# Retention transposes of a 768-token kernel, made per head as products of 64 rows with half the identity

## The reference

```python
def _attn_ref(q, k, v):                      # B=2, H=8 heads, S=768, D=64
    gamma = 1.0 - 2.0 ** (-5.0 - np.arange(H))
    for t in range(S):
        state = gamma[None, :, None, None] * state + np.einsum('bhd,bhe->bhde', k[:, :, t], v[:, :, t])
        y[:, :, t] = scale * np.einsum('bhd,bhde->bhe', q[:, :, t], state)

def _moe_ref(x, U, V, w_ch1, w_ch2):         # x: (2, 768, 512), U: (768, 32), V: (32, 768)
    xt = x.transpose(0, 2, 1)
    h = xt @ U @ V
    u = x + h.transpose(0, 2, 1)
    ch = np.maximum(u @ w_ch1, 0.0) @ w_ch2
    return u + ch

def _moe2_ref(x, w_in, w_spatial, b_spatial, w_out):
    h = np.maximum(x @ w_in, 0.0)            # halves u and v; v is normalised over its channels
    v_s = np.einsum('ts,bsd->btd', w_spatial, v_n) + b_spatial[None, :, None]
    return (u * v_s) @ w_out
```

## Time and profile before

| what | value |
|---|---|
| time, median of 3 runs | 467.19 us (467.06 to 469.72) |
| the profiled execution's own time | 468.86 us |
| its span on the core | 466.9 us |
| TensorE busy | 458.2 us, 98% of the span |
| VectorE busy | 351.3 us, 75% |
| ScalarE busy | 253.6 us, 54% |
| granted TensorE clock, mean | 0.998 of full |

### The profile page before, as it was taken

One profiled execution on the slowest core, in us unless ns is written; L12 is line 12 of the kernel. 1 busy time (PEld: TensorE's weight loads), 2 busy tenths in 40 slices (PEclk: granted clock), 3 DMA queues, 4 the chain that ended last, 5 costly groups with the idle time before them and its releaser, 6 DMA issues.

```text
span 466.9 us, 8670 instructions
## 1 busy us (share of the span) xinstructions
PE 458.2 (98%) x3128; PEld 409.0 (88%) x3128; DVE 351.3 (75%) x772; ACT 253.6 (54%) x592; POOL 48.1 (10%) x52
## 2 busy tenths in 40 slices
PE   8899999999999999999999999999999999999995
PEld 4788898899999999888888999988888789999995
DVE  4788879977889978874855976765813998895783
ACT  1666756546667655843464655733523765564451
POOL 2178970000000000000100000000100001000000
PEclk9999999999999999999999999999999999999999
DMA  8989801433332343201220343302105002041003
GB/s 275 406 298 333 298 3 46 136 135 136 135 126 92 127 137 97 94 24 66 91 91 1 102 130 115 108 1 91 45 1 202 1 0 93 0 155 71 0 1 136
DMA packets 20889, 51.36 MB, mean 110 GB/s; under 512 B 1520, under 2 KB 3952, under 8 KB 19568
## 3 DMA queue, kind: packets, MB, share of 16 engines
q1 hardware_dynamic: 20432, 50.29, 31.3%
q10 hardware_dynamic: 416, 0.53, 0.4%
HBM read 47.66 MB, written 3.15 MB: 109 GB/s over the span
## 4 chain that ended last, share of the span: by engine, by line
PE 94%; DVE 2%; DMA 2%; ACT 1%; issue 0%; DVEq 0%
PE bank L1615 10%; PE bank L1613 10%; PE bank L1616 9%; PE bank L1594 9%; PE bank L1596 9%; PE bank L1597 8%; PE bank L1719 3%; PE bank L1721 3%; PE bank L1722 3%; PE bank L1460 3%; PE bank L1654 2%; PE bank L1653 2%; PE bank L1655 2%; PE bank L1505 2%; PE bank L1499 2%; PE bank L1737 2%
## 5 line engine op out<-in xcount | busy, mean ns | idle before, releaser
L1594 PE MATMUL bank<-bh,w1c 128*128 128x256 f32 x336 | 94.7, 282 | 0.3 <-DVE hl L1099 0.3
L1597 PE MATMUL bank<-bh,w1c 128*128 128x256 f32 x336 | 94.7, 282 | 0.0
L1596 PE MATMUL bank<-bl,w1c 128*128 128x256 f32 x336 | 94.6, 282 | 0.0
L1615 PE MATMUL bank<-hl,w2h 128*128 128x512 f32 x192 | 75.9, 395 | 0.0
L1613 PE MATMUL bank<-hh,w2h 128*128 128x512 f32 x192 | 75.8, 395 | 0.0
L1616 PE MATMUL bank<-hh,w2l 128*128 128x512 f32 x192 | 74.7, 389 | 0.0
L1594 PEld LDWEIGHTS bank<-bh,w1c 128*128 128x128 f32 x336 | 63.5, 189 | 7.0 <-issue 0.5
L1091 DVE TENSOR_TENSOR c<-bank,p 128x256 f32<-128x256 f32 x72 | 30.4, 423 | 51.1 <-PE bank L1597 29.8
L1596 PEld LDWEIGHTS bank<-bl,w1c 128*128 128x128 f32 x336 | 63.4, 189 | 5.4
L1597 PEld LDWEIGHTS bank<-bh,w1c 128*128 128x128 f32 x336 | 63.4, 189 | 0.0
L672 ACT ACTIVATE p<-bank 128x256 f32<-128x256 f32 x72 | 27.5, 381 | 45.4 <-PE bank L1597 44.3
(11 more groups left out here) (179 smaller groups left out, 948.3 us busy)
## 6 DMA issues: line engine op xcount, KB each, us to landing
w1raw<-w SPq DMA_DIRECT2D x24, 512.0 KB, 5.3
w2raw<-w SPq DMA_DIRECT2D x24, 512.0 KB, 4.1
att<-attn SPq DMA_DIRECT2D x7, 1152.0 KB, 7.8
att<-attn SPq DMA_DIRECT2D x10, 384.0 KB, 5.7
out_T<-stage SPq DMA_DIRECT2D x7, 384.0 KB, 2.5
wsp_raw<-w_sp SPq DMA_DIRECT2D x1, 2304.0 KB, 9.1
winraw<-w_in SPq DMA_DIRECT2D x4, 512.0 KB, 4.9
tab<-decay SPq DMA_DIRECT2D x7, 258.0 KB, 5.0
```

What stands on the lines that cost most here:

```text
L1594: mm(o, w1c[k][:, 0, q, s], bh[:, q, c, :], start=(opens and c == 0), stop=False, skip_group_check=True)
L1596: mm(o, w1c[k][:, 0, q, s], bl[:, q, c, :], start=False, stop=False, skip_group_check=True)
L1597: m = mm(o, w1c[k][:, 1, q, s], bh[:, q, c, :], start=False, stop=(c == 1), skip_group_check=True)
L1615: mm(ch_ps[c][:, :], w2h[h][:, s], hl[k][:, h, :], start=False, stop=False, skip_group_check=True)
```

## The change

For items 0 to 6 `turn(i, 0)` and `turn(i, 1)` are replaced by `turn_heads(i)`. It goes through the six chunks, and in each takes the heads one after the other: 64 rows of `xT` (one head's channels) as weights, 128 columns, times the 64 x 64 block of the identity on the same partitions. Head 0 writes `t_ps[0]` (bank 5), head 1 writes `t_ps[1]` (bank 7), 64 columns for each chunk. These are plain float32 products and not the instruction's transpose form. Both `t_done` signals come at the last chunk. The wait for `u_done` (bank 7 has been read by `u_add`) stands ahead of the first product. `xn_copy` and `xn_rest` take a head over all six chunks instead of three chunks with both heads. Item 7 keeps its transposes.

```diff
+        def t_part(i, g):
+            e = DH if i < NI - 1 else P
+            return t_ps[g][:, 0:GW].rearrange("p (c e) -> p c e", e=e)
+
+        def xn_part(t, i, g, s):
+            if i < NI - 1:
+                return t[:, :, s, g * DH:(g + 1) * DH]
+            return t[:, g * G:(g + 1) * G, s, :]
...
             def xn_copy(i, g):
                 act.wait_ge(t_done, 2 * i + g + 1)
-                nc.scalar.activation(xn[:, g * G:(g + 1) * G, 0, :],
-                                     t_ps[g][:, 0:GW].rearrange("p (c e) -> p c e", e=P),
-                                     ACT.Copy).then_inc(xn_hi, 1)
+                nc.scalar.activation(xn_part(xn, i, g, 0), t_part(i, g), ACT.Copy).then_inc(xn_hi, 1)
...
             def xn_rest(i, g):
                 dve.wait_ge(xn_hi, 2 * i + g + 1)
-                nc.vector.tensor_tensor(xn[:, g * G:(g + 1) * G, 1, :],
-                                        t_ps[g][:, 0:GW].rearrange("p (c e) -> p c e", e=P),
-                                        raw(xn)[:, g * G:(g + 1) * G, 0, :], ALU.subtract).then_inc(xn_lo, 1)
+                nc.vector.tensor_tensor(xn_part(xn, i, g, 1), t_part(i, g), xn_part(raw(xn), i, g, 0),
+                                        ALU.subtract).then_inc(xn_lo, 1)
...
+            def turn_heads(i):
+                pe.wait_ge(xt_done, 2 * i + 1)
+                pe.wait_ge(eye_loaded, 16)
+                if i:
+                    pe.wait_ge(u_done, 2 * i - 1)
+                for c in range(NC):
+                    if c == G:
+                        pe.wait_ge(xt_done, 2 * i + 2)
+                    for a in range(2):
+                        h = slice(a * DH, (a + 1) * DH)
+                        m = mm(t_ps[a][:, c * DH:(c + 1) * DH], xT[i % 2][h, c * P:(c + 1) * P], ident[h, h],
+                               start=True, stop=True)
+                        if c == NC - 1:
+                            m.then_inc(t_done, 1)
...
             for i in range(1, NI):
                 scores(i, 0)
-                turn(i - 1, 0)
-                turn(i - 1, 1)
+                turn_heads(i - 1)
```

## The result

| | before | after |
|---|---|---|
| median | 467.12 us | 471.97 us |
| lowest to highest | 466.68 to 469.72, 4 runs | 471.59 to 472.97, 4 runs |
| the profiled execution's own time | 468.86 us | 472.97 us |
| its span | 466.9 us | 470.5 us |

The ratio is 1.0102, with a 95% interval of 1.0088 to 1.0116: the change makes the kernel 4.85 us slower. The forecast was 3.6 us slower.

The account below looks back on a forecast made before the run. TensorE was taken to bound the kernel, busy throughout six iterations. 6 x (0.49 for the products + 0.09 for `down`) + 0.1 for `u_done` = 3.6 us on the 467.19 median gave 470.8 us, range 469.4 to 472.6.

Parts of the forecast that it names:

- The added step: TensorE, last scores to first kv: 12 product pairs at 0.112 us replace the transposes, 1.50 against 1.01, +0.49 us an iteration.
- kv's own border: TensorE's step from kv's last start (45.98) to the next step (46.13), taken as 0.15 us behind the new products.
- Rival (a): Products by heads on TensorE: the moving side sets the pace, 0.058 us a pair; 466.6 to 467.2 us, chance 0.12.
- (c): Rival: load and matmul of a pair don't overlap, 0.16 us a pair; 474.2 us, chance 0.04.
- The wait of `down`: TensorE's `down` waits for VectorE's rest, which ends 0.81 us later: +0.09 us of new wait an iteration.
- `u_done`: TensorE's earlier wait for VectorE's addition, with 0.18 us of cover less the signal's way: 0.1 us for all six iterations.
- the sentence on the length of `decay_q`: On VectorE ahead of `u_done`: where `decay_q` is long, DVE can be up to 0.1 us late.
- Item 0: Turned while TensorE waits for a mask copy anyway: nothing added; without that cover 0.49 us more.
- The forecast's own terms: From 6 x 0.46 without a new wait (469.9 us) to 6 x 0.7 (471.4 us); forecast's chance 0.70.
- rival (b): Chain copy, rest, `down` outgrows its cover: over 1% slower; with runs of 64 slowing copies, 472.2 us; chance 0.14.
- the range: Whole kernel: 469.4 to 472.6 us, leaving out (a), (c) and the far half of (b).
- The chance of 0.20 for over 1% slower: Whole kernel above 471.9 us: made up of (b), (c) and a little of the forecast.

Follow-up runs that it names:

- The first experiment: The changed kernel with each product by heads moving 128 columns instead of 64, same weights: 471.95 us, ratio 1.0098 to the kernel before.
- the second: The changed kernel with each product by heads taking only 64 of a chunk's 128 tokens as weights, bank 5 cleared at the start: 467.91 us, ratio 1.0014.
- transposes late: The kernel before with its transposes kept, but u_done awaited ahead of the first transpose and both t_done signals at the last: 467.73 us, ratio 1.0007.
- Two executions with quarters: The changed kernel with each product cut into two 64 x 64 ones: 470.53 us; the same with decay_q moved behind mask_a(i, 0): 471.33 us.

## Why the prediction was right, and where it was off

*The added step.* The prediction took 0.112 us for a pair, from the loads, and +0.49 for the interval. Measured is 0.111 to 0.112 and an interval of 1.48, +0.47. By the starts of the records the first of the eleven steps is 0.06 and not 0.112, and the border to kv 0.21 and not the 0.15 that was taken from kv's own border; the two cancel. Counted back from the ends of the records, as the prediction did with kv's 0.22, both are as predicted. The first experiment (moving columns doubled, nothing changes) and the second (weight columns halved, the step halves) show that the load is the cause. Rival (a) is dead, and (c) with it: load and moving side do overlap.

*The wait of `down`.* Predicted 0.09, measured 0.10 (0.30 against 0.20 at that border), and isolated with the transposes in place.

*`u_done`.* This is the term that was mis-sized. The prediction put 0.1 us on it for all six iterations together, from 0.18 us of cover and a DVE that "can be up to 0.1 late". It measured 1.2: 1.01 + 1.36 - 2 x 0.58. The profile counts 0.7 of that as waiting. It counts from the end of the last scores record, 0.27 us behind its start, where the first product otherwise starts after 0.11; that is another 0.3. The rest is that behind each of the two waits the 24 records take 1.28 instead of 1.18 us from first start to last. The step of the argument that failed is the sentence on the length of `decay_q`: it took the lengths of before, 0.83 to 1.2 us in these iterations, as fixed. They depend on how much of a GpSimd instruction is still to run when `decay_q` starts, and the change shifts VectorE against GpSimd, which is busy in nearly all of the last two iterations. Where item 6 is turned 0.46 us were left before and 1.19 after, and the 1.15 us of before became 1.86. With iterations of 7.38 and 7.42 us (transposes late, weights halved) the same `decay_q` took 0.94 and 0.87, and nothing waited for `u_done`; so the size of this term is in part chance. In the iteration that turns item 1 it was another lateness: `decay_q` has its 0.83 us but starts 0.24 us late, at 22.05, behind an idle time that the profile puts down to issue, so that the first addition ends at some 23.46, and the first product starts 0.47 us behind the scores instead of 0.11. Why `decay_q` starts late there stays open. With 1.2 instead of 0.1 the sum is 6 x 0.58 + 1.2 = 4.7, the measured value. The prediction calls itself wrong if `u_done` becomes a wait, and it became one: the added step and the wait of `down` held, this mechanism did not.

*Item 0* cost next to nothing, as said: its second half started on ScalarE's copy and the next scores still waited 0.32 us for the mask copy (0.66 before). From the first scores to these it is 16.64 - 13.62 = 3.02 us, against 2.95 before.

*The chances.* The forecast's own terms reached to 471.4 and the measured 471.97 lies beyond them, in what was left to rival (b), whose mechanism (the copies' chain growing through runs of 64) did not happen: two copies take 0.87 us, two rests 1.02, as before. That the range held the time, in the room of a rival that did not happen, is luck. The chance of 0.20 for over 1% slower is what came, with 1.0102 and an interval that reaches down to 1.0088.

## What to carry to other kernels

Half the rows or half the moving columns don't make a product cheaper when its weights keep their width: with 128 float32 columns of weights, a pair of products with 64 moving columns costs as much as one with 128, and the transpose form needs one record of 128 columns for each chunk where the products need two pairs at the same pace. When a change brings a wait forward, look at every occurrence of the instruction ahead of the releaser: which other engine makes it long, and where that engine's instructions will lie after the change, decide, not its length in one place. When several signals are merged into the last one, walk the chain behind it to the next join; here the chain grew by more than its 0.28 us of cover, and 0.1 us of wait was left.

## What the runs showed of the hardware beyond that

Four quarter-array products start together: 48 float32 records with 64 x 64 weights in 0.71 us.

Two executions with quarters stopped TensorE for 1.5 and 0.6 us, and 1.3 and 0.7 us, with "issue" as the only reason, with 48 records in an item where the change has 24 and with the DMA engines busy at a share of 0.79 or more. None of the traces with 24 records shows it there. Each kernel has one trace, and the cause stays open: no run tests whether the instructions came late.

In the wait of 1.8 us in the kernel with GpSimd's rests moved (no matmul between 75.3 and 77.1), the granted clock fell to half, 1.2 GHz, and came back only some 3 us later (stretches of TensorE: borders, length, busy time, records, granted clock, share of the DMA engines, GB/s):

```profile
75.00:77.10 2.10, 0.33 (x3) 0.92 0.00 0
77.10:78.00 0.90, 0.85 (x4) 0.50 0.00 0
...
80.00:81.00 1.00, 1.00 (x9) 0.90 0.00 0
```

So that wait cost 1.8 us and, by an estimate from these rows, some 1.5 more: TensorE was busy through 3 us at half of the clock. The stretch from the first transpose of item 7 to the last matmul bears it out: 399.7 us here and 396.4 in the change, 3.3 longer.
